# Attention with packed keys, a gated layer and a second layer on one Trainium2 core: the first softmax's row sums applied after the packed product, and the start of the kernel reordered

## The reference

```python
pp  = softmax(P K^T / 8) V            # 32 packed rows per head
x   = softmax(Q pp^T / 8) pp          # 576 tokens of 512 per batch
xn  = x / sqrt(mean(x*x) + 1e-6) * g
y   = (silu(xn W_gate) * (xn W_val)) W_out        # 512 -> 1536 -> 512
h   = y W_in;  out = (max(h,0) + alpha*min(h,0)) W_out2   # 512 -> 2048 -> 512
```

## Time and profile before

| what | value |
|---|---|
| median of 3 runs | 1549.82 us (1549.81 to 1552.16) |
| profiled execution | 1551.79 us, of which the span of the trace is 1550.0 us |
| TensorE busy | 1537.6 us, 99% |
| VectorE, ScalarE, GpSimd busy | 712.3, 434.5, 195.9 us (46%, 28%, 13%) |
| chain that ended last | TensorE 95%, VectorE 3%, ScalarE 1% |
| prologue, until the tile of batch 0 starts | 35.08 us |
| DMA in the prologue | 97% of the 16 engines' time |

### The profile page before, as it was taken

The page is one execution under the profiler, slowest core; times in us unless marked ns, Lnnn a source line. Parts: engine busy times, 40 slices in busy tenths (PEclk is TensorE's granted clock), DMA queues, the critical chain, the costliest instruction groups (busy, mean ns, idle before and its releaser), DMA issues.

```text
span 1550.0 us, 23589 instructions
## 1 busy us (share of the span) xinstructions
PE 1537.6 (99%) x9460; PEld 1265.2 (82%) x9460; DVE 712.3 (46%) x1195; ACT 434.5 (28%) x761; POOL 195.9 (13%) x185
## 2 busy tenths in 40 slices
PE   8999999999999999999999999999999999999999
PEld 3888888787888888798888888888888888888887
DVE  5765555546455555543343333333343333333333
ACT  3545353454444354422111111111111111111111
POOL 2710000000000000064171002020202002020000
PEclk9999999999999999999999999999999999999999
DMA  9222212021121210044200000010100000010000
GB/s 354 83 65 69 67 65 66 25 71 41 65 67 65 66 64 6 17 149 149 102 35 28 27 20 34 0 54 0 54 0 27 27 23 31 0 54 0 27 1 27
DMA packets 53563, 82.35 MB, mean 53 GB/s; under 512 B 16240, under 2 KB 25456, under 8 KB 53104
## 3 DMA queue, kind: packets, MB, share of 16 engines
q1 hardware_dynamic: 48592, 72.37, 13.8%
q10 hardware_dynamic: 4896, 8.92, 1.5%
HBM read 59.25 MB, written 22.02 MB: 52 GB/s over the span
## 4 chain that ended last, share of the span: by engine, by line
PE 95%; DVE 3%; ACT 1%; issue 1%; POOL 0%; DVEq 0%; POOLq 0%; ACTq 0%
PE psum L675 30%; PE psum L677 29%; PE psum L676 29%; PE psum L811 3%; PE psum L773 1%; PE psum L947 1%; PE psum L713 1%; PE psum L728 1%; PE psum L761 0%; PE psum L698 0%; PE psum L780 0%; DVE act L1408 0%; DVE h_lo L1411 0%; DVE e L1282 0%; DVE e L1296 0%
## 5 line engine op out<-in xcount | busy, mean ns | idle before, releaser
L1484 DVE TENSOR_TENSOR h_lo<-g,h_hi 128x512 fp32r<-128x512 f32 x144 | 104.9, 729 | 472.5 <-ACT h_hi L1191 472.5
L1191 ACT CAST h_hi<-g 128x512 fp32r<-128x512 f32 x144 | 89.4, 621 | 633.7 <-PE psum L677 600.3
L675 PE MATMUL psum<-an_hi,m_hi 128*128 128x288 f32 x768 | 237.8, 310 | 2.1 <-DVE an_lo L1352 1.4
L676 PE MATMUL psum<-an_hi,m_lo 128*128 128x288 f32 x768 | 226.5, 295 | 0.0
L677 PE MATMUL psum<-an_lo,m_hi 128*128 128x288 f32 x768 | 226.2, 295 | 0.0
L675 PE MATMUL psum<-h_hi,ow_hi 128*128 128x512 f32 (+2 forms) x480 | 184.1, 384 | 0.7 <-DVE h_lo L1411 0.7
L677 PE MATMUL psum<-h_lo,ow_hi 128*128 128x512 f32 (+2 forms) x480 | 177.6, 370 | 0.0
L676 PE MATMUL psum<-h_hi,ow_lo 128*128 128x512 f32 (+2 forms) x480 | 177.6, 370 | 0.0
L675 PEld LDWEIGHTS psum<-an_hi,m_hi 128*128 128x128 f32 x768 | 144.6, 188 | 24.7 <-issue 13.3
L676 PEld LDWEIGHTS psum<-an_hi,m_lo 128*128 128x128 f32 x768 | 144.9, 189 | 4.8
L1440 DVE TENSOR_TENSOR act_sb<-act_sb,psum 128x288 f32<-128x288 f32 x168 | 75.7, 451 | 151.1 <-PE psum L677 134.7
(11 more groups left out here) (150 smaller groups left out, 2391.4 us busy)
## 6 DMA issues: line engine op xcount, KB each, us to landing
k_sb<-k_t SPq DMA_DIRECT2D x16, 576.0 KB, 5.2
q_sb<-q_t SPq DMA_DIRECT2D x8, 1152.0 KB, 5.4
xs_raw<-y_mid SPq DMA_DIRECT2D x9, 1024.0 KB, 5.2
out_t<-o_sb ACTq DMA_DIRECT2D x34, 256.0 KB, 2.0
v_sb<-v_s SPq DMA_DIRECT2D x8, 1024.0 KB, 5.8
gv_sb<-w_gv SPq DMA_DIRECT2D x4, 1536.0 KB, 19.2
w_raw_front<-w SPq DMA_DIRECT2D x10, 512.0 KB, 3.6
y_mid<-y_low SPq DMA_DIRECT2D x7, 512.0 KB, 2.8
```

The lines of the kernel that those rows point to most:

```text
L675: nc.tensor.matmul(dst, w_hi, hi, start=start, stop=False)
L676: nc.tensor.matmul(dst, w_lo, hi, start=False, stop=False)
L1191: nc.scalar.copy(h2_hi[:, f % 2, :], g32[:, f % 2, :]).then_inc(g_hi_done, 1)
L1484: nc.vector.tensor_tensor(h2_lo[:, s, :], g32[:, s, :], h2_hi[:, s, :].bitcast(F32), ALU.subtract).then_inc(g_lo_done, 1)
```

## The change

Five things change.

1. The first softmax's probabilities are no longer divided by their row sums. `norm` ends with the reciprocal, and DVE's `packed` multiplies `pp` by it while it copies, in two instructions, one for each head group. In batch 0 each group has a PSUM bank, and the copy of the first starts when its 40 matmuls are done. `turn_a` waits for `exp1_done`. Its pieces are regrouped: piece 0 is chunks 0 to 3 of group 0, piece 1 the same of group 1, piece 2 the last chunk of both. DVE now copies pieces 0 and 2, ACT piece 1. Both norms and the copy of piece 0 stand on DVE at `(0, "between", 5)`, piece 2 at `(0, "within", 6)`. Piece 2 on TensorE waits for DVE's copy of piece 0.
2. The fillers are half as wide and counted anew. `gram0` goes ahead of `fold1` on TensorE, `fold1` behind `rsqrt0` on ACT.
3. SP's first load is the keys; p is loaded by ACT's queue.
4. In batch 0 the mean is taken by two products that accumulate, without DVE's sum L1319; one table load on ACT is left out there. In the tile of batch 0 the second exponential of batch 1 (`probs`) moves from before `h_hi` of block 11 to behind it.
5. The activations of batch 0 have four buffers instead of three. POOL waits for the first `an_lo` before it splits its first part of W_out.

```diff
-SLOTS, WIDE_SLOTS = 3, 2
+SLOTS, WIDE_SLOTS, FIRST_ACTS = 3, 2, 4
 DVE_PLACES = {
-    (0, "between", 5): ["turn_a1"], (0, "within", 7): ["packed"],
+    (0, "between", 5): ["norm0", "norm1", "turn_a0"], (0, "within", 6): ["turn_a2"],
+    (0, "within", 7): ["packed"],
 ACT_PLACES = {
-    (0, "between", 5): ["turn_a0"], (0, "within", 6): ["turn_a2"],
-    (0, "within", 8): ["packed"], (0, "after", 11): ["probs"], (0, "between", 11): ["silu"],
+    (0, "between", 5): ["turn_a1"], (0, "within", 8): ["packed"],
 SECOND = {
-    "DVE": {(0, "between", 2): ["max0", "max1"], (0, "between", 3): ["norm0"], (0, "after", 4): ["norm1"]},
+    "DVE": {(0, "between", 2): ["max0", "max1"]},
+    "Activation": {..., (0, "between", 11): ["probs", "silu"]},
 LATER = {
-    "DVE": {(0, "between", 2): ["max0"], (0, "after", 3): ["max1"], (0, "within", 5): ["norm0", "norm1"]},
+    "DVE": {(0, "between", 2): ["max0"], (0, "after", 3): ["max1"]},
+    "Activation": {..., (0, "after", 11): ["probs"], (0, "between", 11): ["silu"]},
-FILLERS = {"scores0": (3, EARLY_BANK), "scores1": (1, EARLY_BANK), "turn_a01": (4, EARLY_BANK),
-           "packed": (1, LATE_BANK), "turn_packed": (1, LATE_BANK), "tokens0": (1, LATE_BANK),
-           "fold1": (2, LATE_BANK), "gram0": (1, LATE_BANK)}
+FILLERS = {"scores0": (5, EARLY_BANK), "turn_a01": (3, EARLY_BANK), "fold0": (2, LATE_BANK), "gram0": (4, EARLY_BANK),
+           "fold2": (2, LATE_BANK), "tiles": (4, LATE_BANK)}
...
         def at_ps(c, t):
-            if t == 2:
-                return psum[:, 4 if first(c) else 2, 0:GROUPS * P]
-            return psum[:, 2 + t, :]
+            bank = [5, 6, 4][t] if first(c) else [2, 3, 2][t]
+            return psum[:, bank, 0:GROUPS * P] if t == 2 else psum[:, bank, :]
...
             def turn_a(c, t):
+                pe.wait_ge(exp1_done, GROUPS * c + min(t + 1, GROUPS))
                 if t == 0:
-                    pe.wait_ge(a_normed, GROUPS * (c + 1))
...
                 if t == 2 and c > 0:
-                    pe.wait_ge(at_act, 2 * c + 1)
+                    pe.wait_ge(at_dve, 2 * c + 1)
...
             def mean(c, h):
+                    nc.tensor.matmul(mean_ps(c, h), mean_w[:], w[:, 0, :], start=True, stop=False)
+                    nc.tensor.matmul(mean_ps(c, h), mean_w[:], w[:, 1, :], start=False, stop=True).then_inc(mean_mm, 1)
...
             def turn_a(c, t):
+                dve.wait_ge(at_mm, 3 * c + t + 1)
+                if t == 0:
+                    if c > 1:
+                        dve.wait_ge(y_stored, 32 * (c - 1))
+                    nc.vector.tensor_copy(a_t[:, 0:CHUNKS - 1, 0:P],
+                                          at_ps(c, 0).rearrange("p (j n) -> p j n", n=P)).then_inc(at_dve, 1)
+                else:
+                    nc.vector.tensor_copy(a_t[LAST:P, CHUNKS - 1, :], at_ps(c, 2)[LAST:P, :]).then_inc(at_dve, 1)
...
             def packed(c):   
-                nc.vector.tensor_copy(flat(pp[:]), pp_ps).then_inc(pp_copied, 1)
+                dve.wait_ge(rcp1_done, 2 * c + 2)
+                for e in range(2):
+                    dve.wait_ge(pp_mm, 2 * c + (e + 1 if first(c) else 2))
+                    nc.vector.tensor_scalar(pp[:, e, :], pp_ps(c, e), rcp1[:, e:e + 1], None, ALU.mult).then_inc(pp_copied, 1)
```

More of the change, by code:

```diff
@@ L87 @@
            (0, "ready", 2): ["scores1_ready"], (0, "after", 2): ["scores1"]},
[2 rows of a table removed]
+    "DVE": {(0, "between", 2): ["max0", "max1"]},
+    "Activation": {(0, "between", 1): ["scores0"], (0, "between", 2): ["scores1"], (0, "after", 3): ["exp0", "exp1"],
+                   (0, "between", 11): ["probs", "silu"]},
 }
@@ L92 @@
     "PE": {},
-    "DVE": {(0, "between", 2): ["max0"], (0, "after", 3): ["max1"], (0, "within", 5): ["norm0", "norm1"]},
-    "Activation": {(0, "between", 0): ["scores0"], (0, "after", 1): ["scores1"], (0, "after", 4): ["exp0", "exp1"]},
+    "DVE": {(0, "between", 2): ["max0"], (0, "after", 3): ["max1"]},
+    "Activation": {(0, "between", 0): ["scores0"], (0, "after", 1): ["scores1"], (0, "after", 4): ["exp0", "exp1"],
+                   (0, "after", 11): ["probs"], (0, "between", 11): ["silu"]},
 }
@@ L361, in build @@
         y_stored = sem("y_stored")
-        rest_out = [sem(f"rest_out{n}") for n in range(SLOTS)]
+        rest_out = [sem(f"rest_out{n}") for n in range(FIRST_ACTS)]
         rest_in = [sem(f"rest_in{n}") for n in range(3)]
@@ L946, in keep_busy @@
                 for _ in range(count):
-                    nc.tensor.matmul(psum[:, bank, :].rearrange("p (a n) -> p a n", n=P), mean_w[:],
-                                     ident[:].unsqueeze(1).to_broadcast([P, BANK // P, P]), start=True, stop=True)
+                    nc.tensor.matmul(psum[:, bank, 0:2 * P].rearrange("p (a n) -> p a n", n=P), mean_w[:],
+                                     ident[:].unsqueeze(1).to_broadcast([P, 2, P]), start=True, stop=True)
             pe.wait_ge(consts_set, 2)
             for name in ("scores0", "scores1", "turn_a01", "turn_a2", "packed", "turn_packed", "tokens0", "fold0", "tokens1",
-                         "fold1", "gram0", "mean0", "fold2", "fold3"):
+                         "gram0", "fold1", "mean0", "fold2", "fold3"):
                 if name in FILLERS:
@@ L1021, in scores_exp, with turn_a @@
                                      accum_out=sum1[:, g:g + 1]).then_inc(exp1_done, 1)
-            def turn_a(c, t):
-                if t == 0 and c > 1:
+            def turn_a(c):
+                if c > 1:
                     act.wait_ge(newton_step, 3 * c + 3)
                     act.wait_ge(y_stored, 32 * (c - 1))
-                act.wait_ge(at_mm, 3 * c + t + 1)
-                rows = slice(0, P) if t == 0 else slice(LAST, P)
-                dst = a_t[rows, 2 * t:min(2 * t + 2, CHUNKS), :]
-                nc.scalar.copy(dst.rearrange("p j n -> p (j n)"), at_ps(c, t)[rows, :]).then_inc(at_act, 1)
+                act.wait_ge(at_mm, 3 * c + 2)
+                nc.scalar.copy(a_t[:, 0:CHUNKS - 1, P:2 * P], at_ps(c, 1).rearrange("p (j n) -> p j n", n=P)).then_inc(at_act, 1)
             def packed(c):
@@ L1049, in rsqrt @@
                 n = c + halves.stop if first(c) else c + 2
-                nc.scalar.preload_act_table_set("natural_log_exp_and_others")
+                if not first(c) or halves.start > 0:
+                    nc.scalar.preload_act_table_set("natural_log_exp_and_others")
                 act.wait_ge(mean_copied, 2 * c + halves.stop)
@@ L1174, in rest_tile @@
                 out_of_tile(BATCH)
+            act.dma_start(p_sb[:], p_t[0].rearrange("p (q k) -> p q k", q=PAIRS)).then_inc(p_in, 16)
             nc.scalar.preload_act_table_set("natural_log_exp_and_others")
-            for name in ("exp0", "exp1", "turn_a0", "turn_a2", "packed", "probs0", "fold0", "fold1", "probs1",
-                         "rsqrt0", "silu", "split0", "fold2", "fold3"):
+            for name in ("exp0", "exp1", "turn_a1", "packed", "probs0", "fold0", "probs1",
+                         "rsqrt0", "fold1", "silu", "split0", "fold2", "fold3"):
                 beside(0, name)
```

98 lines of the change are left out of this document (49 added, 49 removed), and 1 row of the table SECOND.

## The result

The changed kernel takes **1557.15 us** (median of 5 runs, 1556.79 to 1557.57), the kernel before 1551.57 (5 runs, 1549.81 to 1552.16): the ratio is 1.0039, 95% interval 1.0025 to 1.0054. Forecast was 1553.4, 1549.3 to 1555.9. So the direction was right and the size was not: it is slower by more than the range held. The profiled executions are 1557.15 us (span 1555.3) against 1551.79 (span 1550.0). One run of the kernel before in a later round took 2552.09 us at a mean granted clock of 0.556, and is left out of every ratio.

The account below looks back on a forecast made before the run. TensorE was taken as the bound, busy without a gap from 115 us. From the profiled 1551.79 us the terms gave 1551.79 - 2.7 - 1.4 - 1.15 + 6.9 = 1553.4 us, range 1549.3 to 1555.9.

Parts of the forecast that it names:

- start of the tile: Prologue: the tile of batch 0 starts at 32.4 instead of 35.08, 2.7 us saved (bounds 1.2 and 3.6).
- tile of batch 0: Waits in that tile: mean 0.1, norm 0.25, `h_lo` 0.8, in all 1.15 us saved (bounds 2 saved, 1 lost).
- term of batches 2 to 7: Last transposes wait for DVE's copy, 1.15 us in each of six batches: 6.9 lost (bounds 4.2 and 8.4).
- clock in its first block: First block of batch 0's tile at full clock: takes 1.6 instead of 3.02, 1.4 us saved (bounds 0 and 1.5).
- the start, as far as the second scores: Prologue: maxima at 8.15, `packed` at 12.25, second scores at 14.55; 4.2 us won up to there.
- the first part of w_gv ... I take 17.85: Prologue: this load, which `fold0` needs, moves by 0.46 at most from 18.0; `fold0` goes from 19.32 to 17.85.
- where the clock falls: Rival, prologue: clock falls in a 2.2 us pause between `tokens1` and `gram0`, tile 1.5 later, about 1555.2 us; chance 0.18.
- the last transposes then wait for DVE, by 0.4: Tile of batch 0: the norm's wait goes, but this 0.4 wait comes; 0.25 us saved with handovers.
- The copy wasn't in time: Rival, bank 2 at the last transposes: DVE's copy is in time, no wait, 1546.5 us; chance 0.12.
- half hidden: Rival, last transposes: small instructions run in the shadow of `h_lo`, wait about 0.7 us, 1550.7 us; chance 0.15.
- No overlap on DVE: Rival, DVE ahead of the last transposes: no overlap between instructions, wait 1.38 us, 1554.8 us; chance 0.05.

Follow-up runs that it names:

- kernel 1: Changed kernel with DVE's copy of piece 0 put ahead of `h_lo`, the norms staying behind it: 1548.31 us, ratio 0.9989 to the kernel before.
- kernel 2: Changed kernel with the last transposes of batches 1 to 7 in bank 3, which ACT's copy frees: 1548.13 us, ratio 0.9986 to the kernel before.
- (8): The kernel before, unchanged, run once more for a second trace: 1549.46 us, span 1547.7.
- kernel 5: Changed kernel with eight fillers instead of two ahead of `fold0`: 1556.93 us, ratio 1.0044 to the kernel before.
- kernel 4: Changed kernel with p loaded first on SP's queue again, before the keys: 1557.82 us, ratio 1.0052 to the kernel before.
- kernel 9: The kernel before with the new fillers alone, `gram0`'s four in the late bank: 1550.27 us, ratio 1.0006 to the kernel before.
- kernel 3: Changed kernel with the two norms behind DVE's copy of piece 0, the copy still behind `h_lo`: 1553.27 us, ratio 1.002 to the kernel before.
- (6): Changed kernel with `tokens1` ahead of `fold0` on TensorE in the prologue: 1554.77 us, ratio 1.0025 to the kernel before.
- kernel 10: Kernel 7 with three fillers ahead of `tokens1` and three instead of two ahead of `fold0`: 1544.81 us, ratio 0.9966 to the kernel before.
- kernel 7: Changed kernel with both the last transposes in bank 3 and `tokens1` ahead of `fold0`: 1545.85 us, ratio 0.9974 to the kernel before.

## Why the prediction was right and wrong

The direction was right, and by the mechanism that was named; the size was not. The steps that failed are two. The start of the tile was put 2.7 us earlier and came 1.35 earlier: w_gv's first part, taken at 17.85, landed at 18.85, and the clock fell in that wait. The tile of batch 0 was put 1.15 shorter and came 0.33 longer: its last transposes waited 1.40 and not 0.4, and two waits came that the sum had at nothing. The term of batches 2 to 7 was right in kind and 0.65 too small. The sum, term by term, from the traces of before and after:

| term | forecast | measured |
|---|---|---|
| start of the tile | -2.7 | -1.35 |
| clock in its first block | -1.4 | -1.34 |
| second block to batch 2's transposes, without their wait | -1.15 | +0.33 |
| waits of batches 2 to 7 | +6.9 | +7.55 |
| behind them | 0 | +0.1 |
| sum | +1.65 | +5.3 |

The third is (148.35 - 37.38) - (149.49 - 40.07) - 1.22, the second block starting at 40.07 and 37.38. The fourth is 1.22 for batch 2 and, for the five batches from there, (591.77 - 148.35) - (586.58 - 149.49) = 6.33.

**Right: what decides.** A wait for DVE's copy behind `h_lo` and the norms in each of the six batches, with nothing to catch it up; kernels 1 and 2 show it by taking it away. The per batch price was 1.15 against 1.22. The handover from the copy to the transposes, taken as 0.05, is 0.14 in batch 2; the rest of the order came 0.02 early. Another 0.05 a batch, 6.33/5 less 1.22, is not placed.

**Right: the start, as far as the second scores.** Forecast 14.55, measured 14.5, though two errors cancel there: the maxima were earlier than I said (7.71 for 8.15) and the way from them longer. The keys, issued 0.46 sooner, landed 0.33 sooner than in the trace of before (5.02 and 6.76).

**Right with luck: the clock in the first block.** It is 1.00 in after, as forecast, but in the second trace of before (8) it is 1.00 too. The 1.34 is there because the trace of before happened to be one of the upper group.

**Wrong: "the first part of w_gv ... I take 17.85".** That is the step that failed in the prologue. Issued 0.3 sooner, it landed 0.9 later than in the trace of before (0.6 than in its second trace), so `fold0` started at 18.99. The argument that saturated DMA engines let it move by 0.46 at most looked at one side alone, at how much sooner it can land; the lower bound of the term, 1.2, had the outcome. TensorE came to the second scores 4.2 us sooner than before and then stood 2.69 in front of a transfer.

**Wrong: where the clock falls.** The rival put the pause between `tokens1` and `gram0`. It came before `fold0`, in the wait for w_gv, and cost at `tokens1`: 1.32 instead of 0.72 us for its records, as the row at 20.01 and the same 16 records of kernel 5 at 20.09 show it. Kernel 4, whose clock didn't fall there, starts the tile at 32.89 where after has 33.73. The step from `fold0` to the tile can be taken from both: forecast 14.55, in kernel 4 14.03 (from 18.86), in after 14.74. So the start fell short by 1.14 through w_gv and by 0.71 through the clock, and 0.52 came back because the rest of the way was shorter than I had put it: 1.33, of the 1.35 of the table. This rival happened in its mechanism, had 0.18, and its price of 1.5 was too high; the first block stayed at full clock.

**Wrong: "the last transposes then wait for DVE, by 0.4".** In batch 1 they wait as in the others, and more. Timeline of after:

```profile
55.20 1.29 POOL L621 TENSOR_TENSOR m_lo<-m_raw,m_hi 128x512 fp32r<-128x512 f32 x1
...
55.41 1.40 DVE L1424 TENSOR_TENSOR h_lo<-act,h_hi 128x288 fp32r<-128x288 f32 x1 [0.50 <-ACT h_hi L1124]
...
57.23 0.67 DVE L1262 COPY a_t<-psum 128x512 f32<-128x512 f32 x1
...
58.05 0.41 PE L715 MATMUL psum<-ident,a_sb 128*128 128x128 f32 x2 [1.25 <-DVE a_t L1262]
```

`h_lo` of 128x288, whose median is 0.46 us, takes 1.40 beside POOL's subtraction, so the copy comes only at 57.23. In kernel 2, without the wait, the transposes come 1.24 after the start of `h_lo` (54.87 and 56.11), here 2.64: a wait of 1.40, not 0.4. The rows to see it were there: the earlier trace rows give 1165 ns as the longest of line 1249 against a median of 520.

The other half of this term's miss are two waits that the sum had at nothing. Timeline of after:

```profile
38.28 1.28 POOL L621 TENSOR_TENSOR m_lo<-m_raw,m_hi 128x512 fp32r<-128x512 f32 x1
...
38.99 0.89 DVE L1424 TENSOR_TENSOR h_lo<-act,h_hi 128x288 fp32r<-128x288 f32 x1 [2.56 <-ACT h_hi L1124]
...
136.22 0.40 PE L678 MATMUL psum<-an_hi,m_hi 128*128 128x288 f32 x1 [0.17 <-DVE act_sb L1453]
```

The first is the same kind. `h_lo` takes 0.89 beside POOL's subtraction, where it took 0.57 in the trace of before. DVE's next product is later by that, with it ACT's cast and its copy of the scores, and TensorE loses 0.31 us between 39.80 and 41.95; in kernel 2 `h_lo` took 1.12 there and TensorE lost 0.56. The second is in the tile of batch 1: DVE's product before the row at 136.22 starts 0.37 later against TensorE's matmuls than in before, and TensorE loses 0.39. All ten traces with the change have this wait, both of before and kernel 9 don't; what holds that product up isn't shown. What was to be saved was saved, and a little more: 0.65 at the norm, 0.88 at `h_lo` and 0.20 at the mean, where the second trace of before has no wait, so against that one nothing is saved. 1.41 + 0.31 + 0.39 - 0.65 - 0.88 - 0.20 is 0.38, and the table has 0.33.

**The rivals.** The copy wasn't in time, and not half hidden; kernels 1 and 3 show the orders on DVE that each would have taken, changed by hand, and kernel 2 another bank. No overlap on DVE: no, the small instructions start 0.08 before the end of the one ahead, and `h_lo` to the first norm 0.08 as well. The Trainium skill (VectorE: DVE Perf Modes) has, beside the drain, a section "Two Vector instructions with no wait between them", by which only held instructions wait for the end of the one ahead. The rows at 147.01 and 147.27 agree with that section, so the page, read whole, didn't speak for this rival as the prediction had it.

**The range.** All three misses, 1.35, 1.48 and 0.65, point to the slow side. They are 3.5 us together, and the range had 2.5 above the forecast. Each term came out within its own bounds; the range took in the waits' bounds and the clock's rival, but not both with a late w_gv and a slower tile of batch 0. That a start moved forward meets the same transfers and POOL's work at another moment touches several terms, and I had added them as if they were apart.

## What to carry to other kernels

When a step is moved to another engine's list, count what stands ahead of it there at that moment, and look for who waits at the other end; here the copy behind `h_lo` cost 8.8 to 9.0 us more than the copy ahead of it or a bank that another engine frees. This prologue, in front of a late transfer, gained 2.4 us by an order in which the work that doesn't need the transfer comes first (6), while the 4.2 us of shorter steps ahead of it had left 1.35. Look at TensorE's pauses whenever fillers are cut: in kernel 9 fewer fillers gave nothing, and in kernel 10, with a few more, the runs are 0.6 us apart instead of 3.0. And where the runs of a kernel fall in two groups, find out of which group a trace is before its terms are summed.

## What the runs showed of the hardware

- The subtraction `h_lo` of 128x288 took 1.40 us beside a GpSimd subtraction that ran from 55.20 to 56.49, against a median of 0.46. From 38 to 81 us in after nine `h_lo` ran beside a GpSimd subtraction, product or cast, and each ended 0.30 to 0.33 us behind the end of the one that had started before it, after 0.60 to 1.50 us; alone they took 0.41 to 0.46. The Trainium skill (SBUF — State Buffer, "SBUF: two separate sides") says that DVE, in an operation with two SBUF inputs, and a GpSimd operation that reads SBUF lock one another out of a port pair that they share, for the whole instruction; the rows agree.
- From the end of DVE's copy (147.52 + 0.69) to TensorE's transposes it is 0.14 us in after and 0.15 in kernel 3.
- The granted clock fell to half (1.2 GHz) behind stretches in which TensorE was busy for 0.31 of 3 us (after), 1.09 of 3 (kernel 7), 1.95 of 4.3 (kernel 9) and 1.43 of 3 (kernel 5), and it stayed up in kernel 10 with 2.48 of 3. But in the wait for w_gv, from 16 to 19 us, it fell behind 0.49 (kernel 1) and 0.55 of 3 (kernel 3) and stayed up behind 0.65 (kernel 2) and 0.82 (kernel 4), which is less than the 1.09 of kernel 7. So the busy share of a stretch doesn't settle it. The same kernel before was at half from 31.22 to 38.05 us in one trace and from 30.87 to 34.29 in the other.
- Behind the fall in the wait for w_gv (19.67 to 23.09 in after) the tile started 0.71 us later, counted from `fold0`, than in kernel 4, where the clock stayed up.
- The first part of w_gv landed at 18.56 to 19.37 us in the ten kernels with the change or most of it and at 17.98 to 18.29 in the other three traces; with p back on SP's queue it was 18.73. The second part followed 3.83 or 3.84 us behind it in the ten and 4.37 to 5.29 in the three. The cause is open.
